# Linear attention and two MLPs on one core: the first phase's six masked levels as a loop on TensorE

## What is computed

```python
for t in range(S):                                   # attention
    state = alpha[:, :, t, :, None] * state + np.einsum('bhd,bhe->bhde', k[:, :, t], v[:, :, t])
    y[:, :, t] = np.einsum('bhd,bhde->bhe', q[:, :, t], state)
u = x + (x.transpose(0, 2, 1) @ U @ V).transpose(0, 2, 1)        # x = attention's output, heads side by side
x2 = u + np.maximum(u @ w_ch1, 0.0) @ w_ch2
h = np.maximum(x2 @ w_in, 0.0); u, v = h[..., :d_ff // 2], h[..., d_ff // 2:]
v_s = np.einsum('ts,bsd->btd', w_spatial, normalized(v)) + b_spatial[None, :, None]
out = (u * v_s) @ w_out
```

## Time and profile before

| | |
|---|---|
| time, median of 3 runs (lowest, highest) | 798.35 us (797.75, 798.8) |
| the profiled execution: its time, its span | 794.5 us, 792.7 us |
| TensorE busy, share of the span | 724.8 us, 91% |
| DVE, ACT, POOL busy | 341.1, 332.4, 223.8 us |
| granted TensorE clock, mean of the span | 0.991 |
| packets of the instruction queue q8, whole span | 85 (1.39 MB) |

### The profile page before, as it was taken

How to read it: one execution, slowest core, us unless ns; L and a number is a source line. 1 busy time by engine, 2 the same in 40 slices (tenths; PEclk the granted TensorE clock), 3 DMA queues, 4 the chain that set the end, 5 groups by cost and what they waited for, 6 DMA issues and landing times.

```text
span 792.7 us, 25598 instructions
## 1 busy us (share of the span) xinstructions
PE 724.8 (91%) x11408; PEld 684.7 (86%) x11408; DVE 341.1 (43%) x593; ACT 332.4 (42%) x574; POOL 223.8 (28%) x152
## 2 busy tenths in 40 slices
PE   1356978997999998999999999999999999999998
PEld 1345867987999997999999989998998999999998
DVE  4674256553656554556546231212431431531531
ACT  5447364641744642644643432232422422413411
POOL 6456038211115212016122043232132033033021
PEclk9999989998999999999999999999999999999999
DMA  9211460131140112140100023214003003001001
GB/s 258 98 44 57 151 171 3 37 98 37 37 131 5 38 48 87 37 131 4 38 33 3 2 90 120 63 48 150 1 11 110 0 1 120 0 0 60 0 0 60
DMA packets 15700, 47.25 MB, mean 60 GB/s; under 512 B 1680, under 2 KB 8080, under 8 KB 15088
## 3 DMA queue, kind: packets, MB, share of 16 engines
q1 hardware_dynamic: 15600, 45.73, 18.5%
HBM read 36.29 MB, written 9.44 MB: 58 GB/s over the span
## 4 chain that ended last, share of the span: by engine, by line
PE 82%; issue 4%; DVE 2%; ACT 1%; DMA 1%; POOL 1%; SPq 0%; DVEq 0%; POOLq 0%
PE HB L779 24%; PE ZB L779 9%; PE ZB L856 6%; PE ZB L858 6%; PE ZB L857 6%; PE SB L779 6%; PE SB L692 4%; PE ZB L892 3%; PE HB L892 3%; PE SB L892 2%; PE SB L761 2%; PE HB L897 2%; PE ZB L897 2%; PE SB L770 1%; DMA x2s<-in_w 1%
## 5 line engine op out<-in xcount | busy, mean ns | idle before, releaser
L1064 ACT ACTIVATE hid_hi<-HB 128x384 fp32r<-128x384 f32 x96 | 47.2, 492 | 170.3 <-PE HB L779 170.1
L1285 DVE SCALAR_TENSOR_TENSOR hid_lo<-HB,hid_hi 128x384 fp32r<-128x384 f32 x96 | 53.5, 557 | 149.3 <-ACT hid_hi L1064 148.3
L779 PE MATMUL HB<-uh,w1h 128*128 128x384 f32 x288 | 104.0, 361 | 2.5 <-DVE ul L1281 2.5
L856 PE MATMUL ZB<-hid_hi,w2h 128*128 128x384 f32 x288 | 99.3, 345 | 0.0
L779 PE MATMUL HB<-ul,w1h 128*128 128x384 f32 x288 | 97.5, 339 | 1.4 <-issue 1.4
L779 PE MATMUL HB<-uh,w1l 128*128 128x384 f32 x288 | 97.3, 338 | 0.0
L858 PE MATMUL ZB<-hid_lo,w2h 128*128 128x384 f32 x288 | 97.3, 338 | 0.0
L857 PE MATMUL ZB<-hid_hi,w2l 128*128 128x384 f32 x288 | 96.9, 337 | 0.0
L692 PEld LDWEIGHTS SB<-Qd,K 112*32 112x32 f32 x4032 | 43.7, 117 | 45.8 <-issue 33.5
L616 POOL TENSOR_TENSOR gl<-gated,gh 128x384 fp32r<-128x384 f32 x32 | 32.4, 1013 | 178.5 <-ACT gh L1079 178.5
L692 PE MATMUL SB<-Qd,K 112*32 112x32 f32 x4032 | 49.2, 206 | 35.8 <-issue 19.3
(11 more groups left out here) (212 smaller groups left out, 1480.1 us busy)
## 6 DMA issues: line engine op xcount, KB each, us to landing
Q<-in_q SPq DMA_DIRECT2D x8, 672.0 KB, 7.6
K<-in_k SPq DMA_DIRECT2D x7, 672.0 KB, 4.7
AL<-in_al SPq DMA_DIRECT2D x7, 672.0 KB, 5.9
Vt<-in_v SPq DMA_DIRECT2D x8, 576.0 KB, 9.5
x2s<-in_w SPq DMA_DIRECT2D x12, 384.0 KB, 7.8
mid<-x2s SPq DMA_DIRECT2D x8, 576.0 KB, 3.9
x<-mid SPq DMA_DIRECT2D x4, 1152.0 KB, 5.6
out<-o_sb SPq DMA_DIRECT2D x24, 192.0 KB, 1.8
```

Source lines behind the costliest of these rows:

```text
L779: last = nc.tensor.matmul(dst, weights(x, w), moving(y, m), start=(n == 0 and x == y == 0), stop=(n == total - 1 and y == 1))
L856: nc.tensor.matmul(bank, w2h[:, i, cols], hi, start=(i == 0), stop=False)
L1064: nc.scalar.activation(hid_hi[:, i % HID, :], HB[i % 2][:, 0:TILE], ACT.Relu).then_inc(h_hi, 1)
L1285: nc.vector.scalar_tensor_tensor(hid_lo[:, i % HID, :], HB[i % 2][:, 0:TILE], 0.0, hid_hi[:, i % HID, :].bitcast(F32), ALU.max, ALU.subtra ...
```

## The change

TensorE runs levels 0 to 5 of batch 0 as a loop over n, whose body is one level of group 0 and one of group 1. For a body that doesn't change with n, each group uses one spread buffer (Qd[0]) and one score bank (SB[1] of its workspace) in all six levels. Levels 6 on stay written out, the two groups in turn (LAST_STEPS). All engines follow: no stagger, level by level, group 0 then group 1. Other parts:

- ScalarE spreads level n of a group when its scores of level n - 1 are done.
- VectorE doesn't make all totals first: take, K and the first total of a group, then its odd Q product, then the other totals. The even Q product of level 1 goes to GpSimd. A K product waits for the take of its level, since the bank is used again.
- Two of a group's four square copies go to VectorE (behind level 7), the other two stay on ScalarE but move to KV_STEP, behind the casts of weight pieces 3 and 4 (and, for group 1, of 5).
- GpSimd splits no weights among its Q products: all low parts come behind the last one. SPLITS and SPLIT_V of ScalarE and VectorE move later.
- SyncE issues the first three weight pieces ahead of the values.
- Semaphore counts change with that (k_ready starts at 1, ad_copied counts two for each group). The attention of later batches keeps its two buffers and its order.

The core of the diff:

```diff
-FIRST_STEPS = [(g, k - STAGGER * g) for k in range(STEPS + STAGGER * (GROUPS - 1)) for g in range(GROUPS)
-               if 0 <= k - STAGGER * g < STEPS]
-SPLITS = {(0, 5): [0], (0, 6): [1, 2], (0, 7): [3], (1, 6): [4], (1, 7): [5]}
-SPLIT_V = {(1, 2): 0, (1, 3): 1, (1, 4): 2}
+LAST_STEPS = [(g, n) for n in range(MASKED, STEPS) for g in range(GROUPS)]
+SPLITS = {(1, MASKED): [0], (0, LEVELS - 1): [1], (1, LEVELS - 1): [2], (0, T_STEP): [3], (1, T_STEP): [4],
+          (0, KV_STEP): [5]}
+SPLIT_V = {(1, LEVELS - 1): 0, (0, KV_STEP): 1, (1, KV_STEP): 2}
...
+            for n in range(STAGE):
+                load_piece(n)
             for g in range(GROUPS):
                 load_values(0, g)
...
+            for g, w in enumerate(spaces):
+                pool.wait_ge(ld_al[g], 16)
+                pool.wait_ge(qd_ready[g], 2)
+                nc.gpsimd.tensor_tensor(even(Q[g][:, :], 1), even(Q[g][:, :], 1), even(w.tot[1], 1), ALU.mult
+                                        ).then_inc(q_even[g], 1)
+            for n in range(2, LEVELS):
+                for g in range(GROUPS):
                     scale_q(0, g, n)
-                for m in SPLITS.get((g, n), []):
-                    split_low(m)
-            for n in range(W1_PIECES, W1_PIECES + STAGE):
+            for n in range(W1_PIECES + STAGE):
                 split_low(n)
...
+            def first_level(g, n):
+                w = space(0, g)
+                pe.wait_ge(ld_k[g], 16)
+                pe.wait_ge(qd_ready[g], 2 * n + 2)
+                pe.wait_ge(k_ready[g], n + 1)
+                square_scores(level_bank(w, n, True), w.K, w.Qd[0]).then_inc(score_done[g], 1)
...
-            for g, n in FIRST_STEPS:
+            pe.wait_ge(zeroed_s, 4)
+            with pe.Fori(0, MASKED) as n:
+                for g in range(GROUPS):
+                    first_level(g, n)
+            for g, n in LAST_STEPS:
                 att_step(0, g, n, True)
...
+            def first_spread(g, n):
+                if n > 1:
+                    act.wait_ge(q_ready[g], n - 1)
+                act.wait_ge(score_done[g], n)
+                spread(0, g, n, True)
...
+            for n in range(MASKED):
+                for g in range(GROUPS):
+                    if n == 0:
+                        att_start(0, g, True)
+                    else:
+                        first_spread(g, n)
+            for g, n in LAST_STEPS:
                 att_step(0, g, n, True)
                 for m in SPLITS.get((g, n), []):
                     split_high(m)
...
+                if a == 0 and n < MASKED:
+                    dve.wait_ge(a_dve[g], n + 1)
                 dve.wait_ge(score_done[g], SCORES * a + (SCORES if n == LEVELS - 1 else n + 1))
...
+            first_level(0)
+            totals(0, 0, range(1, LEVELS - 1))
+            first_level(1)
+            for n in range(1, MASKED):
+                for g in range(GROUPS):
+                    for piece in range(vector_pieces(n)):
+                        att_piece(0, g, n, piece, True)
+                    if (g, n) == (0, 1):
+                        totals(0, 1, range(1, LEVELS - 1))
+            for g, n in LAST_STEPS:
                 for piece in range(vector_pieces(n)):
                     att_piece(0, g, n, piece, True)
+                if n == LEVELS - 1:
+                    square_copies(g, QUARTERS[2:])
                 if (g, n) in SPLIT_V:
                     split_v(SPLIT_V[g, n])
```

More of the change, by code:

```diff
@@ L280, in workspace @@
             small, o = place(f"small{name}", [ROWS, FLAT // 4], o)
-            w.Qd = [None] * 2
-            for i in range(2):
+            w.Qd = [None] * (2 if at_k is None else 1)
+            for i in range(len(w.Qd)):
                 w.Qd[i], o = place(f"Qd{i}{name}", [ROWS, UNITS, 2, HALF], o)
@@ L364, in build @@
         q_ready = [sem(f"q_ready{g}") for g in range(GROUPS)]
+        q_even = [sem(f"q_even{g}") for g in range(GROUPS)]
         k_ready = [sem(f"k_ready{g}") for g in range(GROUPS)]
@@ L532, in _ @@
             sp.dma_start(V_in[:, :], v_w).then_inc(ld_uv, 16)
-            for n in range(W1_PIECES):
+            for n in range(STAGE, W1_PIECES):
                 load_piece(n)
@@ L658, in _, with square_scores @@
         def _(pe):
+            def square_scores(bank, keys, queries):
+                for u in range(UNITS):
+                    for j in range(NBLK):
+                        first_key = u * CH + j * BLOCK
+                        last = nc.tensor.matmul(bank[j * BLOCK:(j + 1) * BLOCK, u * BLOCK:(u + 1) * BLOCK],
+                                                keys[:, first_key:first_key + BLOCK],
+                                                queries[:, u, :, j * HB32:(j + 1) * HB32], start=True, stop=True)
+                return last
+            def first_level(g, n):
[4 more added lines that the diff above has]
+                square_scores(level_bank(w, n, True), w.K, w.Qd[0]).then_inc(score_done[g], 1)
             def att_step(a, g, n, first):
@@ L687, in att_step @@
                     if n < MASKED:
[L688 to L691, removed]
-                                last = nc.tensor.matmul(bank[j * BLOCK:(j + 1) * BLOCK, u * BLOCK:(u + 1) * BLOCK],
-                                                        w.K[:, first_key:first_key + BLOCK],
-                                                        w.Qd[n % 2][:, u, :, j * HB32:(j + 1) * HB32],
-                                                        start=True, stop=True)
-                        last.then_inc(score_done[g], 1)
+                        square_scores(score_bank(w, n), w.K, w.Qd[n % 2]).then_inc(score_done[g], 1)
                     elif n == MASKED:
@@ L930, in _, with spread @@
         def _(act):
-            def spread(a, g, n):
+            def spread(a, g, n, first):
                 for hh in range(2):
@@ L973, in att_step @@
                     act.wait_ge(score_done[g], SCORES * a + n)
-                    spread(a, g, n + 1)
+                    spread(a, g, n + 1, False)
                 if n == LEVELS - 2:
@@ L1000, in att_step @@
                         last.then_inc(a_act[g], 1)
-                if n == KV_STEP and not first:
-                    square_copies(a, g)
+                if n == KV_STEP:
+                    square_copies(a, g, QUARTERS[:2] if first else QUARTERS)
                 if n == Y_STEP - 1:
@@ L1183, in take, with att_start, totals @@
                 nc.vector.copy_predicated(dst, m, src).then_inc(a_dve[g], 1)
-            def att_start(a, g, first):
+            def att_start(a, g):
                 dve.wait_ge(ld_al[g], 16 * (a + 1))
-                if not first:
-                    pa, pg = before(a, g)
-                    dve.wait_ge(aux_done[pg], AUX * pa + AUX_KV)
-                    dve.wait_ge(q_ready[pg], (LEVELS - 1) * (pa + 1))
-                for i in range(LEVELS - 1):
+                pa, pg = before(a, g)
+                dve.wait_ge(aux_done[pg], AUX * pa + AUX_KV)
+                dve.wait_ge(q_ready[pg], (LEVELS - 1) * (pa + 1))
+                totals(a, g, range(LEVELS - 1))
+            def totals(a, g, which):
+                for i in which:
                     if i:
@@ L1252, in att_piece, with square_copies @@
                     last.then_inc(state_step[g], 1)
+            def square_copies(g, rows):
+                w = space(0, g)
+                dve.wait_ge(a_dve[g], MASKED)
+                dve.wait_ge(zeroed_a[g], 1)
+                for r in rows:
+                    last = nc.vector.tensor_copy(w.A[r, :, :, r], w.Ad[r, :, :, :])
+                last.then_inc(ad_copied[g], 1)
             def split_v(part):
```

94 lines of the change are left out of this document (49 added, 45 removed).

## The result

The changed kernel took 785.12 us, the median of 4 runs (783.49 to 789.09), against 798.35 before: 13.2 less, ratio 0.984 (95% interval 0.980 to 0.988). More executions put the difference a little lower. Over all experiments the changed kernel was executed 33 times with a median of 786.0 (781.1 to 793.5) and the kernel before 91 times with 796.5 (789.7 to 802.2; two executions of 1029 and 1771 us are left out): 10.5 us.

The account below looks back on a forecast made before the run. TensorE, 91% busy, bounds the kernel; the end is tied to group 0's last product plus 10.64 of loads. That product 5.0 earlier (84.0 against 88.98), off the 798.35 median, gives 793.4 us; range 788.5 to 800.0.

Parts of the forecast that it names:

- the rest: Work outside the main chain: weight pieces and decays shift, and all behind the first w2 piece is unchanged, moving with G.
- G: End of group 0's last output product in batch 0: forecast at 84.0 us, 5.0 earlier than 88.98.
- a change of more than 1.5 behind G: Sign against the forecast: time from G to the end changing by more than 1.5 us, which no step provides for.
- Loop: TensorE's six masked levels: five jumps at 0.35 us each, no code fetches inside, about 7 fewer instruction packets.
- Rival D: TensorE's loop doesn't keep its code, each jump fetching its first packet: 6 us slower, 804; chance 0.15.
- Levels: Batch 0's masked levels: level 1 ends on VectorE at 29.2, four rounds of 4.55 follow, last masked scores about 45.
- Square copies: Two square copies of a group on VectorE hold GpSimd by 1.2 us, moving its last Q product's end to 59.5.
- Wait for the w1 pieces: ScalarE idles for w1 loads twice or more between 62 and 70; group 1's first A product starts at 71 to 73.
- Clock: TensorE's tail: clock rises 5.9 us after 71.4, at 77.3, so three A products are slow (5.85) and two fast (2.1).
- Behind G: After group 0's last product: 10.6 us to the first w2 piece, later work unchanged, about 1.5 either way for the clock.

Follow-up runs that it names:

- e11: Kernel before with 126 idle semaphore increments spread over TensorE's idle times in the first phase, shifting later packet cuts: 784.47 us, ratio 0.984 to before.
- e12: Changed kernel with 130 idle increments on TensorE, so later packets are cut as in the kernel before: 790.86 us, ratio 0.992 to before.
- e16: Changed kernel unaltered, run again as a control: 788.40 us, ratio 0.991 to before.
- e5: Changed kernel with GpSimd waiting for group 1's last K product before its first weight split: 789.54 us, ratio 0.988 to before.
- e6: Changed kernel with GpSimd waiting for group 1's last K product and ScalarE's casts of weight pieces 3 to 5 later: 781.18 us, ratio 0.982.

## Why the prediction was wrong, and where it was right

**The step that failed** is the one in the part on the rest: "All work behind the first w2 piece is unchanged and moves with G." The work is unchanged, the time isn't: 692.7 before and 688.1 after from the restart on (means of three and five profiles), and e11 brings it to 685.2 with no part of the change at all. The removed instructions move every later packet against the loads, and in the kernel before two packets that were wanted while a group's loads held the DMA engines, near 180 and near 300 us, cost up to 4.87 and 4.04 us of TensorE and mostly a stretch at the lower clock. The prediction read the packets as a cost of the first phase only. The waits for issue behind 101 us stood in the same trace: 4.87 at 182.6 and 2.86 at 304.4. It named a change of more than 1.5 behind G as what would prove it wrong, and that is what came: 705.6 before and 701.6 after from G to the end, 4.0 less. The result lies 8.3 us under the 793.4 forecast; 4.0 of it is this, 2.7 is how the first few executions fell (13.2 in place of 10.5), and 1.6 isn't located.

**G itself** was right: 84.0 forecast, 83.1 measured in the mean (82.54 in the profile), 4.9 earlier, where 5.0 was forecast. The worth of the whole change with equal cuts behind it isn't that clear: 6.2 us with the cuts of the kernel before (e12 against it), 1.1 with the others (the changed kernel against e11). And G came out right partly by luck, over terms that were off in both directions:

- *Loop.* Right. 0.22 per jump and 0.30 idle, where 0.35 was priced; 8 packets fewer, 7 forecast. Rival D is out: the jumps fetched nothing. D leaned on the rule of the Trainium skill, Runtime: NRT & Kernel Launch, section Instruction fetch mechanics, that a jump out of a window of two pages fetches again. This loop doesn't test that rule: its body is 384 instructions, 192 matmul records with 192 weight loads, one and a half packets, so D's 804 didn't follow from it. The trace that doesn't agree is that of stage two's loop, 684 instructions, with no packet in its last two rounds.
- *Levels.* Mis-sized; the masked scores ended at 48.9, not 45. Level 1 was done on VectorE at 31.6, not 29.2: one wait of 1.85 for GpSimd was counted, the trace has four products of totals that take 2.90, 2.52, 1.73 and 1.83 beside GpSimd's Q products. The four rounds, counted by their ends, took 19.6 in place of 18.2, two of some 5.9 (products of 2.32 and 1.68 in place of 0.95) and two of some 3.9, where K_side's products met nothing; the new wait between take and product costs 0.2 each time.
- *Square copies.* The direction was wrong. They were to hold GpSimd by 1.2. GpSimd, with a Q product and three splits in a row, held the second copy for 7.03 us and so the K product behind it, and that was on the path: group 1's transposes stood 6.42.
- *Wait for the w1 pieces.* Half right. ScalarE was idle for a piece once (2.50), not twice; piece 5's cast came at 72.71 and group 1's first A product at 75.27, 3.9 later than forecast.
- *Clock.* The rise was counted from the A products (71.4 + 5.9 = 77.3). TensorE had worked without a gap since the transposes at 67.8, and the table by stretches has the granted clock at 0.50 up to 73.0 and at 1.00 behind it, ahead of all A products. From 75.27 to 80.07 five of them took 4.8 in place of 7.95, and these 3.2 cancelled most of the lateness.
- *Behind G.* 11.3 to the first w2 piece where 10.6 was forecast, and the restart 13.5 behind G against 12.9: right within 0.7.

The size was also taken off one execution's trace, while executions of the kernel before spread over 12 us (789.7 to 802.2). The first profile before was one with a short second stretch (117.7 us from batch 1's token mixing to batch 2's, 120.6 and 120.7 in the other two).

## What to carry to other kernels

A change in the number of instructions on a long written-out engine moves every later packet of code against the loads, also where nothing was edited; so before crediting a structural change with a gain of a per cent, put the same number of idle instructions into the kernel before, where the engine is idle anyway, and measure that. Look for waits for issue beside full DMA slices in the whole trace, not only in the stage under work: here shifting the cuts by half a packet, in the first phase and behind it, was worth 12.5 us by itself, where the whole change was worth 13.6 on the same chip. And let an engine that has slack wait for the product that is on the path, rather than run several operations in a row ahead of it: here that, with the casts moved, took 8.8 us off.

## What the hardware showed that was not expected

- GpSimd's operations back to back can hold one VectorE operation through all of them: 7.0 us in eleven profiles for a copy of 32x768 that began inside a Q product (1.65 us) with three splits straight behind it (5.32), 7.53 for one product that takes 0.96 alone. The Trainium skill, SBUF — State Buffer, section Who interferes with whom, says that where the two contend, whichever issues first gets the shared pair of ports for the whole instruction and the other blocks. These traces go further, since VectorE did not get its turn between GpSimd's operations. In e5 and e6 the trace agrees: VectorE's copies, cast and product took 1.85 to 2.08 each beside three and four splits in a row. What decides between the two courses isn't known.
- A semaphore increment on TensorE's queue took 0.14 us each, 126 of them 17.64.
- A packet wanted near 180 us with a DMA share of 1.01 to 1.04 in the 2 us ahead left TensorE idle for 3.3 to 4.9 us, against 0.4 to 2.3 where it was cut elsewhere; in five of the six cases the granted clock fell to its lower level for 6.8 us, from inside the wait on, in the sixth for 3.4 behind it.
- The same kernel had 5.3 us idle at 292 to 293 us in two of five profiles (e16 and the first) and at most 1.5 in the other three. Why isn't settled.
